# Gram products in half fills over eight steps, and the numerator of feed-forward layer 0 summed by an adding DMA

## What is computed

```python
k_n = k / (norm(k) + 1e-6)
for t in range(S):
    y[t] = q[t] @ state
    state = state + beta[t] * outer(k_n[t], v[t] - k_n[t] @ state)

# layer 0
h = x @ w_in
P = a[0] + a[1] * h + a[2] * h**2 + a[3] * h**3
Q = 1 + abs(b[0]) * abs(h) + abs(b[1]) * h**2
x = (P / (Q + 1e-6)) @ w_out

# layer 1
h = x @ w_in
g = h * tanh(log1p(exp(min(h, 20))))
out = g @ w_out
```

## Time and profile before

| | |
|---|---|
| runs | 1152.55 us median of 3 (1148.77 to 1155.8) |
| the profiled execution | 1156.6 us, of which the span is 1154.8 us |
| delta rule | 0 to about 305 us |
| layer 0, first to last g_lo | 326.5 to 756.0 us |
| layer 1 | to the end |
| busy, share of the span | PE 90%, DVE 81%, ACT 63%, POOL 16% |
| mean granted clock of TensorE | 0.947 |

### The profile page before, as it was taken

One profiled execution on the slowest core, in us unless ns is written; L12 is line 12 of the kernel. 1 busy time (PEld: TensorE's weight loads), 2 busy tenths in 40 slices (PEclk: granted clock), 3 DMA queues, 4 the chain that ended last, 5 costly groups with the idle time before them and its releaser, 6 DMA issues.

```text
span 1154.8 us, 24086 instructions
## 1 busy us (share of the span) xinstructions
PE 1039.5 (90%) x10274; PEld 823.8 (71%) x10280; DVE 935.9 (81%) x996; ACT 727.5 (63%) x943; POOL 185.2 (16%) x332
## 2 busy tenths in 40 slices
PE   4487788988888999999999999899999999999997
PEld 2365565766666777777877778678888888888886
DVE  4965555456399999999999999999788887878785
ACT  1133434455487787777868778777766767667664
POOL 5088886582000000000000000000000000000000
PEclk6579989799899999999999999999999999999999
DMA  7823434223300010100101002240100101010000
GB/s 173 234 58 99 112 100 126 60 71 113 111 28 28 1 55 1 55 0 0 54 0 55 1 18 96 79 136 1 43 12 1 55 0 54 0 55 1 28 1 28
DMA packets 28192, 61.82 MB, mean 54 GB/s; under 512 B 3648, under 2 KB 11328, under 8 KB 28096
## 3 DMA queue, kind: packets, MB, share of 16 engines
q1 hardware_dynamic: 27584, 59.13, 17.0%
q10 hardware_dynamic: 512, 1.31, 0.5%
HBM read 46.27 MB, written 14.16 MB: 52 GB/s over the span
## 4 chain that ended last, share of the span: by engine, by line
DVE 35%; PE 34%; issue 3%; ACT 2%; DVEq 0%; ACTq 0%
PE o_ps L838 6%; PE o_ps L840 6%; PE o_ps L839 6%; PE h_ps L839 6%; PE h_ps L838 6%; PE h_ps L840 6%; DVE val L1023 5%; DVE val L1042 5%; DVE val L1055 5%; DVE g_lo L1061 5%; DVE den L1015 5%; DVE den L1050 5%; DVE pa L1021 5%; PE h_ps L882 0%; ACT den L902 0%
## 5 line engine op out<-in xcount | busy, mean ns | idle before, releaser
L911 ACT ACTIVATE g_hi<-val 128x1024 fp32r<-128x1024 f32 x96 | 102.0, 1062 | 100.1 <-DVE val L1055 94.0
L838 PE MATMUL o_ps<-g_hi,w_hi_late 128*128 128x512 f32 x288 | 116.7, 405 | 20.8 <-DVE g_lo L1061 20.7
L1055 DVE SCALAR_TENSOR_TENSOR val<-den,val 128x1024 f32<-128x1024 f32 x96 | 117.7, 1226 | 10.3
L838 PE MATMUL o_ps<-g_hi,w_hi_early 128*128 128x512 f32 x288 | 114.5, 398 | 12.8 <-ACT stage L948 9.2
L1061 DVE SCALAR_TENSOR_TENSOR g_lo<-val,g_hi 128x1024 fp32r<-128x1024 f32 x96 | 117.6, 1225 | 1.6 <-ACT g_hi L911 1.5
L838 PE MATMUL h_ps<-x_hi,w_hi_early 128*128 128x512 f32 x288 | 112.9, 392 | 2.0 <-DVE val L1023 2.0
L838 PE MATMUL h_ps<-x_hi,w_hi_late 128*128 128x512 f32 x288 | 112.5, 391 | 1.6 <-DVE w_lo_late L87 1.6
L839 PE MATMUL o_ps<-g_lo,w_hi_late 128*128 128x512 f32 x288 | 113.5, 394 | 0.0
L840 PE MATMUL o_ps<-g_hi,w_lo_early 128*128 128x512 f32 x288 | 113.4, 394 | 0.0
L840 PE MATMUL o_ps<-g_hi,w_lo_late 128*128 128x512 f32 x288 | 113.3, 394 | 0.0
L839 PE MATMUL o_ps<-g_lo,w_hi_early 128*128 128x512 f32 x288 | 113.3, 393 | 0.0
(11 more groups left out here) (114 smaller groups left out, 2226.3 us busy)
## 6 DMA issues: line engine op xcount, KB each, us to landing
w_raw<-w SPq DMA_DIRECT2D x16, 768.0 KB, 5.0
kv_run<-kv_n SPq DMA_DIRECT2D x24, 384.0 KB, 3.7
x_raw<-x_dram SPq DMA_DIRECT2D x12, 768.0 KB, 5.7
kq<-kq_t SPq DMA_DIRECT2D x44, 192.0 KB, 5.1
x_dram<-stage SPq DMA_DIRECT2D x12, 384.0 KB, 4.3
x_dram<-stage SPq DMA_DIRECT2D x6, 768.0 KB, 4.2
out<-stage SPq DMA_DIRECT2D x5, 768.0 KB, 4.1
k_norm<-kv_n SPq DMA_DIRECT2D x4, 768.0 KB, 7.3
```

The lines of the kernel that those rows point to most:

```text
L838: nc.tensor.matmul(dst, hi, rhs_hi, start=first, stop=False)
L911: act_fn(g_hi[:, n % 2], val[:, n % 2], ACT.Copy, scale=-1.0).then_inc(g_hi_ready, 1)
L1055: dve_stt(val[:, e], den[:, e], 2.0, val[:, e], ALU.subtract, ALU.mult).then_inc(g_ready, 1)
```

## The change

It has two independent parts.

*Gram*: a fill is split into its two chunks. Tables say which (fill, chunk) each step does: one per step in tiles 1 to 3; in tile 0 none in steps 0 and 7 and two in steps 3 and 6. A fill is scaled in the step of its second chunk. Both transposes of n_mat stand in step 7 of tile 0 for tile 2 (ahead of the transposes of the inverse), and for tiles 3, 4 and 5 in step 0 of tile 2, 3 and 4, after copy_low.

*Layer 0*: P = (a3 h + a2) h^2 + (a1 h + a0). ScalarE computes both brackets, VectorE multiplies the first by sq, and a DMA of GpSimd adds the product, pa, to val (128 x 1024 fp32, both in SBUF). VectorE's instructions that read h are gone; ScalarE's last read of h sets h_read.

```diff
+GRAM_FIRST = ((), ((0, 0),), ((0, 1),), ((1, 0), (1, 1)), ((2, 0),), ((2, 1),), ((3, 0), (3, 1)), ())
+GRAM = (((0, 0),), ((0, 1),), ((1, 0),), ((1, 1),), ((2, 0),), ((2, 1),), ((3, 0),), ((3, 1),))
...
-                    if tau + 2 < T and 0 <= fill < 4:
-                        gram_fill(tau + 2, fill)
+                    if tau + 2 < T:
+                        for f, c2 in (GRAM if tau else GRAM_FIRST)[s]:
+                            gram_fill(tau + 2, f, (c2,))
...
-                    if tau + 2 < T and 0 <= fill < 4:
-                        scale_gram(tau + 2, fill)
+                    if tau + 2 < T:
+                        for f, c2 in (GRAM if tau else GRAM_FIRST)[s]:
+                            if c2 == 1:
+                                scale_gram(tau + 2, f)
...
-                    if fill == 3 and tau + 2 < T:
-                        turn_n(tau + 2, 0, half_k)
-                    if fill == 4 and tau + 2 < T:
-                        turn_n(tau + 2, half_k, C)
+                    if s == 7 and tau == 0:
+                        turn_n(2, 0, half_k)
+                        turn_n(2, half_k, C)
+                    if s == 0 and tau >= 2 and tau + 1 < T:
+                        turn_n(tau + 1, 0, half_k)
+                        turn_n(tau + 1, half_k, C)
...
+            def numerator(dt, n):
+                e = n % 2
+                pool.wait_ge(line_ready, DT * dt + n + 1)
+                pool.wait_ge(cubic_ready, DT * dt + n + 1)
+                pool.sem_inc(pool_passed, 1)
+                nc.gpsimd.dma_start(val[:, e], pa[:, e], accum_op=ALU.add).then_inc(num_added, 16)
...
                 if layer == 0:
                     act_fn(sq[:, e], h, ACT.Square)
-                    act_fn(den[:, e], h, ACT.Abs, scale=cf[:, 4:5]).then_inc(abs_ready, 1)
                     act_fn(pa[:, e], h, ACT.Identity, scale=cf[:, 3:4], bias=cf[:, 2:3]).then_inc(lead_ready, 1)
+                    if warm:
+                        act.wait_ge(g_lo_ready, DT * dt + n - 1)
+                    act_fn(val[:, e], h, ACT.Identity, scale=cf[:, 1:2], bias=cf[:, 0:1]).then_inc(line_ready, 1)
+                    act_fn(den[:, e], h, ACT.Abs, scale=cf[:, 4:5]).then_inc(h_read, 1)
...
-            def above(dt, n):
+            def cubic(dt, n):
                 dve.wait_ge(lead_ready, DT * dt + n + 1)
-                dve_tt(pa[:, e], pa[:, e], h_ps[e][:], ALU.mult).then_inc(inner_ready, 1)
-                dve.wait_ge(inner_ready, DT * dt + n + 1)
-                dve_stt(val[:, e], pa[:, e], cf[:, 1:2], h_ps[e][:], ALU.add, ALU.mult).then_inc(h_read, 1)
+                dve_tt(pa[:, e], pa[:, e], sq[:, e], ALU.mult).then_inc(cubic_ready, 1)
...
                 dve.wait_ge(rec_ready, DT * dt + n + 1)
-                dve.wait_ge(h_read, DT * dt + n + 1 + 2)
                 if layer == 0:
-                    dve_stt(val[:, e], val[:, e], cf[:, 0:1], rec[:, e], ALU.add, ALU.mult).then_inc(ratio_ready, 1)
+                    dve.wait_ge(num_added, 16 * DT * dt + 16 * n + 16)
                 else:
-                    dve_tt(val[:, e], val[:, e], rec[:, e], ALU.mult).then_inc(ratio_ready, 1)
+                    dve.wait_ge(h_read, DT * dt + n + 1 + 2)
+                dve_tt(val[:, e], val[:, e], rec[:, e], ALU.mult).then_inc(ratio_ready, 1)
```

More of the change, by code:

```diff
@@ L342, in keep_warm, with gram_fill @@
                     nc.tensor.matmul(side_ps[:], busy[:, 0:P], busy, start=True, stop=True)
-            def gram_fill(j, f):
+            def gram_fill(j, f, chunks=range(2)):
                 cp, r = f // 2, f % 2
                 if r == 0:
-                    for c2 in range(2):
+                    for c2 in chunks:
                         pe.wait_ge(kq_loaded[slot(j, 2 * cp + c2)], 32 * (j // RING) + 32)
-                if j >= 2:
+                if j >= 2 and 0 in chunks:
                     pe.wait_ge(gram_used, 4 * j + f)
@@ L360, in gram_fill @@
                                                     start=True, stop=True)
-                last.then_inc(gram_done, 1)
+                if 1 in chunks:
+                    last.then_inc(gram_done, 1)
             def k_state(tau, c, g):
@@ L464, in _ @@
                     q = index(tau, c, g)
-                    fill = s - (1 if tau == 0 else 0)
                     if tau and s == 0:
@@ L777, in feed_forward @@
         h_done, h_read = sem("h_done"), sem("h_read")
-        abs_ready, lead_ready = sem("abs_ready"), sem("lead_ready")
+        line_ready, lead_ready = sem("line_ready"), sem("lead_ready")
+        cubic_ready, num_added = sem("cubic_ready"), sem("num_added")
+        pool_passed = sem("pool_passed")
         exp_ready, clip_ready, one_ready = sem("exp_ready"), sem("clip_ready"), sem("one_ready")
         q_ready, ln_ready, rec_ready = sem("q_ready"), sem("ln_ready"), sem("rec_ready")
-        inner_ready, ratio_ready, unit_ready = sem("inner_ready"), sem("ratio_ready"), sem("unit_ready")
+        ratio_ready, unit_ready = sem("ratio_ready"), sem("unit_ready")
         g_ready = sem("g_ready")
@@ L833, in _ @@
             sp.wait_ge(o_stored, 16 * (2 * T + KT))
+        @block.gpsimd
+        def _(pool):
+            def numerator(dt, n):
[4 more added lines that the diff above has]
+                nc.gpsimd.dma_start(val[:, e], pa[:, e], accum_op=ALU.add).then_inc(num_added, 16)
+            with pool.Fori(0, T // 2) as dt:
+                for n in range(DT):
+                    numerator(dt, n)
         @block.tensor
@@ L894, in _, with front @@
             act_fn = nc.scalar.activation
-            def front(layer, dt, n):
+            def front(layer, dt, n, warm=True):
                 e = n % 2
@@ L961, in two_tiles @@
                     if following is not None:
-                        front(following, dt, n + 1)
+                        front(following, dt, n + 1, not (first and n == 0))
                     if following == 1:
@@ L989, in _ @@
             act.wait_ge(coef_made, 2)
-            front(0, 0, 0)
+            front(0, 0, 0, False)
             logarithm(0, 0, 0)
@@ L1013, in below @@
                 e = n % 2
-                dve.wait_ge(abs_ready, DT * dt + n + 1)
+                dve.wait_ge(h_read, DT * dt + n + 1 + 2)
                 dve_stt(den[:, e], sq[:, e], cf[:, 6:7], den[:, e], ALU.mult, ALU.add).then_inc(q_ready, 1)
-            def above(dt, n):
+            def cubic(dt, n):
                 e = n % 2
                 dve.wait_ge(lead_ready, DT * dt + n + 1)
-                dve_tt(pa[:, e], pa[:, e], h_ps[e][:], ALU.mult).then_inc(inner_ready, 1)
-                dve.wait_ge(inner_ready, DT * dt + n + 1)
-                dve_stt(val[:, e], pa[:, e], cf[:, 1:2], h_ps[e][:], ALU.add, ALU.mult).then_inc(h_read, 1)
+                dve_tt(pa[:, e], pa[:, e], sq[:, e], ALU.mult).then_inc(cubic_ready, 1)
             def clipped(dt, n):
@@ L1039, in ratio, with unit @@
                 dve.wait_ge(rec_ready, DT * dt + n + 1)
-                dve.wait_ge(h_read, DT * dt + n + 1 + 2)
                 if layer == 0:
-                    dve_stt(val[:, e], val[:, e], cf[:, 0:1], rec[:, e], ALU.add, ALU.mult).then_inc(ratio_ready, 1)
+                    dve.wait_ge(num_added, 16 * DT * dt + 16 * n + 16)
                 else:
-                    dve_tt(val[:, e], val[:, e], rec[:, e], ALU.mult).then_inc(ratio_ready, 1)
-            def corrected(layer, dt, n):
+                    dve.wait_ge(h_read, DT * dt + n + 1 + 2)
+                dve_tt(val[:, e], val[:, e], rec[:, e], ALU.mult).then_inc(ratio_ready, 1)
+            def unit(layer, dt, n):
                 e = n % 2
+                dve.wait_ge(rec_ready, DT * dt + n + 1)
                 if layer == 0:
@@ L1052, in corrected @@
                     dve_stt(den[:, e], sq[:, e], 1.0, rec[:, e], ALU.add, ALU.mult).then_inc(unit_ready, 1)
+            def corrected(dt, n):
+                e = n % 2
                 dve.wait_ge(ratio_ready, DT * dt + n + 1)
@@ L1070, in two_tiles @@
                     following = layer if n + 1 < DT else after
[L1071 to L1074, removed]
+                    if layer == 0:
+                        unit(layer, dt, n)
+                        ratio(layer, dt, n)
+                        if following == 0:
+                            cubic(dt, n + 1)
+                        else:
+                            clipped(dt, n + 1)
+                    else:
+                        ratio(layer, dt, n)
+                        if following == 1:
+                            clipped(dt, n + 1)
+                        unit(layer, dt, n)
+                    corrected(dt, n)
                     if following == 0:
@@ L1077, in two_tiles @@
                         low_part(dt, n)
-                        above(dt, n + 1)
                     elif following == 1:
@@ L1097, in _ @@
             dve.wait_ge(coef_made, 2)
+            cubic(0, 0)
             below(0, 0)
-            above(0, 0)
```

## The result

The changed kernel took 1161.74 us (median of 20 runs, 1154.29 to 1170.79) against 1151.89 (20 runs of before on the same chips): ratio 1.0078, 95% interval 1.006 to 1.0097. It is slower, by 9.9 us between the medians: less than 1%, but clear of the scatter. The profiled execution has a span of 1161.5 us, before 1154.8: 6.7 more.

A forecast was written before the change was run, and what follows sets the result against it. Layer 0 was taken as bound by VectorE, layer 1 by TensorE, with 2.9 us spare for tile 5's inverse. Delta rule +21 and layer 0 -12 gave +9 on 1152.55: 1161.5 us, range 1144 to 1200 (the forecast's own 1154 to 1169).

The forecast's parts named there:

- Tile 4, the late inverse: Delta rule: GpSimd's pass for tile 5 starts later, so x_mat comes at 285.4 instead of 269.64, +15.7 us.
- Tiles 2 and 3: Delta rule: later Gram transposes delay x_mat, +2.5 us in tile 3 and half of it, +1.3, in tile 2.
- The restart of TensorE: Delta rule, after tile 4's long wait: warm matmuls at half clock ahead of the solve, +1.5 us (bounds 0 and 2.5).
- Tiles 0 and 1: Delta rule: transposes of tile 2 before x_mat of tile 1 against evener steps, taken as 0 (bounds -4 and +3).
- Layer 0's pace: Feed-forward layer 0: loop through ScalarE's reciprocal and VectorE, 8.2 us, 8.55 with per-tile work against 8.87; -15 us over 47 pairs.
- rival 3: Layer 0 faster: ScalarE's slack is made up and pace falls to TensorE's 8.13 us per pair, total 1141.5 us; chance 0.12.
- The adding DMA: Layer 0: GpSimd's 512 KB add takes 5.5 us of 5.8 free between cubic and ratio, so it is hidden.
- Rival 1: Layer 0: the add is late, at 7 us the loop takes 9.45 us per pair, total 1200 us; chance 0.25.
- Its other form: Layer 0: issuing the add must wait for VectorE's running instruction, so 1.2 us join 5.5, giving 6.7 us.
- Rivals 2 and 4: Layer 0 gains nothing, 1174 us, chance 0.13; GpSimd's pass shortens so the inverse isn't late, 1140 us, chance 0.07.

The follow-up runs named there:

- early5: The changed kernel with whole Gram fills in tile 3 and tile 5's matrix transposed in steps 4 and 5 of tile 3: 1153.6 us, ratio 1.000 to before.
- gram_only: The kernel of before with only the Gram part of the change, layer 0 as before: 1173.29 us, ratio 1.0195.
- first_half: The changed kernel with half fills and late transposes in tile 0 only, whole fills in tiles 1 to 3: 1142.95 us, ratio 0.9927 to before.
- pe_less: `ff_only` without the low part of x in layer 0's hidden products, 30 matmuls per pair instead of 36: undisturbed pairs 8.13 us, layer 0 415.8 us.
- late2: `ff_only` with two GpSimd memsets of a spare buffer before each adding DMA is issued: 1200.84 us (one run), layer 0 472.4 us.
- ff_only: The kernel of before with only the layer 0 part of the change, whole Gram fills kept: 1144.84 us against 1152.45, ratio 0.9925.
- no_add: `ff_only` without the adding DMA, GpSimd only passing the signal: layer 0 408.6 us against 414.3, undisturbed pairs 8.14 us as with it.

## Why the prediction was right, and where it was not
The time (1161.5 forecast, 1161.74 measured) was hit closer than its parts deserve, and that closeness is luck: two terms were too small and one that I had at 0 took about as much off.

- *Tile 4, the late inverse.* Right, in mechanism and size: x_mat came 45.6 us after the first u_blk of tile 4, the sum said 45.4. Against before that is +15.9 (forecast 15.7). `early5` shows the cause.
- *Tiles 2 and 3.* The waits for GpSimd came (2.59 and 5.75 us in the trace). From the first u_blk of the tile to x_mat it is +0.6 and +1.7, where I had +1.3 and +2.5. That the tiles grew by 3.6 and 4.3 is mostly the next point.
- *The restart of TensorE.* This is the term that I under-sized: I counted it once, at 1.5 of at most 2.5 us. From x_mat to the next u_blk it is 3.0, 3.0 and 3.7 us before and 6.0, 5.7 and 5.7 after, at three tile boundaries: +3.0, +2.7 and +1.9, some 8 us. Most of it, 2.4, 2.1 and 1.9, is in the 11 warm matmuls. In `gram_only` and `early5`, too, each of the three boundaries at which x_mat waited for GpSimd has 4.7 to 5.6 us there, also behind the shortest waits of TensorE (3.4 us); in the seven traces without such waits it is 3.0 to 3.9.
- *Tiles 0 and 1.* Taken as 0, the trace shows -5.2, which hid the error above. Whether the half fills take part in it is open (`first_half`); traces with the same code lie up to 10 us apart, so this term can't be read from one pair of traces.
- *Layer 0's pace.* Right: 8.14 against 8.2 for the loop, 8.48 against 8.55 with the work once per tile. The copy-out pair was 1.2 longer, the split of x 1.1, x_lo 0.4; I had 1.2, 1.0 and 0.5. `pe_less` shows that the limit is not TensorE; rival 3 falls with it. Layer 0 gained 14.5 against 15. Its start cost 3.6 us where I had 2.5. So the part is worth about 11 us by the traces; that it alone brought 8.6 us in time lies within its interval.
- *The adding DMA.* Right in outcome: landing 4.6 after issue, 5.2 after cubic, I had taken 5.5 of 5.8. By the Trainium skill ("DMA: Bandwidth & Descriptors", Anatomy of one DMA, for the copy, and "Collectives: The Full Stack", the section on the fold count, for the two reads) the estimate was 4.4; the measured 4.6 agrees. Rival 1 was real as a mechanism: in `late2` the add lands 2.78 + 4.6 = 7.4 us after cubic, for which the rival's sum gives 9.8 per pair, and 9.78 was measured (48 us dearer than before). In the changed kernel it struck two pairs, by 4.64 and 1.12 us, beside transfers of SP and not by VectorE. Its other form, an issue that waits for VectorE's instruction, did not come: the issue took 0.86 us in the median and 1.01 at most, and in `ff_only` it began at 552.24, in the middle of an instruction of VectorE (551.59 to 552.81).
- *Rivals 2 and 4.* No instruction of VectorE stretched (between 410 and 500 us those without a coefficient take 1219 to 1226 ns in the mean where it was 1212 to 1226), and GpSimd's pass kept its 37 and 40.7 us.

## What to carry to other kernels
Before a step is moved later, find the longest serial work that starts behind it, on whatever engine, and count from the new start to the moment of need in the shortest stage; here 2.9 us were spare, and the pass for tile 5 began 18.5 us later, counted from the first u_blk of tile 4 (13.6 us ahead of it before, 4.8 behind it after). Count the restart at every place where TensorE has to wait: here it came back with its clock at the lower level and lost 1.9 to 3.0 us more, after a wait of 3 us as after one of 17. And when the busiest engine of a stage is relieved, write down the loop that is left, since work once per tile then sets the pace only if it stands in that loop: cut into pieces that fit its gaps, it was free.

## What the runs showed of the hardware
An accumulating DMA of 512 KB from SBUF to SBUF, issued by GpSimd, lands 4.5 to 4.6 us after issue in most of 48 cases, and costs GpSimd 0.86 us; with and without it the mean durations on VectorE, ScalarE and TensorE are the same within 5 ns (`ff_only`, `no_add`). Beside four transfers of 768 KB it took 9.9 us, behind a store and a load of x 6.3. I had expected its way to be counted from issue alone: the issue itself follows the end of VectorE's product by 0.56 us, as much as the slack that was left, 0.6. In seven traces with the same code the last x_mat of the delta rule came up to 10 us earlier or later.
